# Expert weights as whole row blocks, rates by tiles, and two transfers' waits on other engines

## The reference, cut to what matters

```python
N, D, E, F = (4608, 512, 8, 1024)
logits = x @ w_gate
e_idx = np.argmax(logits, axis=1)
for e in range(E):
    mask = e_idx == e
    h = np.maximum(x[mask] @ w1[e], 0.0)      # w1[e]: 512 x 1024
    ye = h @ w2[e]                            # w2[e]: 1024 x 512
    out[mask] = gate_w[mask, None] * eom[mask, e, None] * ye
```

## Time and profile before

| | |
|---|---|
| median of 3 runs | 1118.25 us (1117.03 to 1119.43) |
| profiled execution, its own time | 1117.23 us |
| its span | 1115.5 us |
| PE busy | 1050.9 us, 94% |
| DVE, ACT, POOL busy | 581.8, 394.3, 221.9 us |
| mean granted clock of PE | 0.977 of full speed |
| first slot's input transposes | 596.0 us after the span's start |

### The profile page before, as it was taken

How to read it: one execution, slowest core, us unless ns; L and a number is a source line. 1 busy time by engine, 2 the same in 40 slices (tenths; PEclk the granted TensorE clock), 3 DMA queues, 4 the chain that set the end, 5 groups by cost and what they waited for, 6 DMA issues and landing times.

```text
span 1115.5 us, 22675 instructions
## 1 busy us (share of the span) xinstructions
PE 1050.9 (94%) x6189; PEld 873.4 (78%) x6190; DVE 581.8 (52%) x1182; ACT 394.3 (35%) x725; POOL 221.9 (20%) x411
## 2 busy tenths in 40 slices
PE   4899999999999999999965999999999999999695
PEld 3688888888888888888844888888888888888584
DVE  6876767677676767676643434324343332342320
ACT  3443333443343443343421334323333432332321
POOL 2463211212121212121211111111111111111010
PEclk9899999999999999999986999999999999999898
DMA  7542132322122322222003343423334242232100
GB/s 231 185 155 61 55 75 75 75 69 73 49 74 75 76 69 50 70 75 58 20 20 102 118 136 122 135 78 112 113 94 127 82 140 60 81 125 65 29 29 29
DMA packets 57270, 96.71 MB, mean 87 GB/s; under 512 B 15758, under 2 KB 15886, under 8 KB 57232
## 3 DMA queue, kind: packets, MB, share of 16 engines
q1 hardware_dynamic: 47168, 75.60, 22.5%
q0 software_dynamic: 7968, 20.61, 6.2%
q10 hardware_dynamic: 2096, 0.04, 0.1%
HBM read 76.66 MB, written 20.60 MB: 87 GB/s over the span
## 4 chain that ended last, share of the span: by engine, by line
PE 91%; DVE 3%; issue 2%; DMA 2%; ACT 1%; POOL 0%; ACTq 0%; DVEq 0%; SPq 0%; POOLq 0%
PE Y_ps L436 38%; PE H_ps L436 36%; PE T L428 6%; PE S_ps L483 3%; PE X_ps L428 3%; PE X_ps L493 3%; PE S_ps L428 2%; PE L_ps L520 1%; DVE wx L707 1%; DMA stage<-in_moe_w_out 0%; DMA wg<-in_moe_w_output_gate 0%; DMA prob<-x_rows,slot_rec 0%; POOL route_table L1033 0%; DVE dl L707 0%; DVE cen L752 0%
## 5 line engine op out<-in xcount | busy, mean ns | idle before, releaser
L436 PE MATMUL Y_ps<-wx,dh 128*128 (+1 forms) x1216 | 386.1, 399 | 2.4 <-DVE dl L707 2.4
L436 PE MATMUL H_ps<-wx,xh 128*128 (+1 forms) x1216 | 337.2, 399 | 12.2 <-DVE wx L707 8.7
L436 PEld LDWEIGHTS H_ps<-wx,xh 128*128 128x128 f32 x1216 | 225.9, 191 | 56.5 <-issue 11.6
L436 PEld LDWEIGHTS Y_ps<-wx,dh 128*128 128x128 f32 x1216 | 220.1, 188 | 49.3 <-issue 8.1
L436 PE MATMUL Y_ps<-wx,dl 128*128 (+1 forms) x608 | 237.6, 391 | 0.0
L436 PE MATMUL H_ps<-wx,xl 128*128 (+1 forms) x608 | 188.8, 392 | 0.0
L707 DVE TENSOR_TENSOR wx<-stage,wx (+1 forms) x63 | 76.5, 1224 | 157.0 <-ACT wx L660 156.4
L436 PEld LDWEIGHTS H_ps<-wx,xl 128*128 128x128 f32 x608 | 115.0, 189 | 24.7
L436 PEld LDWEIGHTS Y_ps<-wx,dl 128*128 128x128 f32 x608 | 114.1, 188 | 24.8
L739 DVE TENSOR_REDUCE nmax_h<-H_ps 128x1 f32<-128x1024 f32 x36 | 44.1, 1224 | 90.1 <-PE H_ps L436 86.3
L1057 POOL DMA_INDIRECT out<-x,slot_rec x40 | 40.6, 1014 | 215.7 <-ACT x L685 203.7
(11 more groups left out here) (173 smaller groups left out, 1238.2 us busy)
## 6 DMA issues: line engine op xcount, KB each, us to landing
stage<-in_moe_w SPq DMA_DIRECT2D x128, 256.0 KB, 3.0
stage<-in_q SPq DMA_DIRECT2D x36, 256.0 KB, 2.9
stage<-in_k SPq DMA_DIRECT2D x72, 128.0 KB, 3.3
stage<-in_v SPq DMA_DIRECT2D x36, 256.0 KB, 3.2
x_rows<-x SPq DMA_DIRECT2D x36, 256.0 KB, 2.3
stage<-in_moe_w_out SPq DMA_DIRECT2D x4, 512.0 KB, 3.7
stage<-in_moe_w_in SPq DMA_DIRECT2D x3, 512.0 KB, 8.5
slot_rec<-route_table SPq DMA_DIRECT2D x40, 2.0 KB, 1.6
```

The source lines that it names most:

```text
L436: i = pe.matmul(acc[:, c0:c0 + HALF], x[:, kk, :], w(part, kk * cols + c0), start=first and x is hi and part == 0, stop=last and x is lo)
```

## The change

**Row blocks.** The host lays the weights out anew as one input `experts`: for each expert 8 blocks of 128 rows x 1024, first 4 row blocks of `w1`, then 4 pairs of row blocks of `w2`. A piece is one block, loaded by one DMA of 512 KB. H waits for an expert's first 4 pieces, and Y of the slot before waits for all 8 of its expert. Y also starts after the first half of `dl` (`g0_lo`) and waits for the second half (`g1_lo`) in its middle.

**Rates by tiles.** Pieces per slot are 2 for experts of 4 tiles or more, 4 for 2 or 3 tiles, 8 for 1. They reach `(idx + 0.5) * pace` in the middle and `(idx + 1) * pace` at the end of a slot. `i_load` becomes the table of the splits itself, so SP issues a load as soon as the piece 8 before it is split.

**Records by POOL, last waits on SP.** `load_rec` moves to POOL, and SP instead of POOL waits for the landing of the last scatters.

```diff
@@ tables written by DVE
-            link(dve.tensor_scalar(idx, idx, float(SPLIT_RATE), None, ALU.mult))
-            dve.tensor_scalar(mid, idx, float(PIECES), float(PIECES), ALU.min, ALU.add)
-            link(dve.tensor_scalar(idx, idx, 1.0, float(PIECES), ALU.add, ALU.min))
+            dve.tensor_scalar(rate, tiles, 3.5, 2.0, ALU.is_lt, ALU.mult)
+            link(dve.tensor_scalar(rate1, tiles, 1.5, 4.0, ALU.is_lt, ALU.mult))
+            link(dve.scalar_tensor_tensor(rate, rate, 2.0, rate1, ALU.add, ALU.add))
+            link(dve.tensor_tensor(rate1[:, 0:NE - 1], rate[:, 1:], rate[:, 0:NE - 1], ALU.subtract))
+            link(dve.tensor_tensor(wide1[:, :, 0:NE - 1], past[:, :, 0:NE - 1], rate1[:, 0:NE - 1].unsqueeze(1).to_broadcast([1, SLOTS, NE - 1]), ALU.mult))
+            link(dve.tensor_reduce(pace, wide1[:, :, 0:NE - 1], AX.X, ALU.add))
+            link(dve.tensor_scalar(pace, pace, rate[:, 0:1], None, ALU.add))
+            dve.tensor_tensor(mid, idx, pace, ALU.mult)
+            link(dve.scalar_tensor_tensor(idx, idx, 1.0, pace, ALU.add, ALU.mult))
+            link(dve.scalar_tensor_tensor(mid, pace, 0.5, mid, ALU.mult, ALU.add))
+            dve.tensor_scalar(idx, idx, float(PIECES), None, ALU.min)
+            link(dve.tensor_scalar(mid, mid, float(PIECES), float(PIECES), ALU.min, ALU.add))
...
-            link(dve.tensor_scalar(least[:, 0:SLOTS], mid, float(-PIECES), None, ALU.add))
-            link(dve.tensor_tensor(least, least, first, ALU.max))
-            link(dve.tensor_tensor(least, least, till, ALU.min))
             dve.tensor_copy(i_split[:, :], till)
-            dve.tensor_scalar(i_load[:, :], least, limit8, None, ALU.min).then_inc(slots_set, 1)
+            dve.tensor_scalar(i_load[:, :], till, limit8, None, ALU.min).then_inc(slots_set, 1)
@@ SP
-                sp.dma_start(buf[:, 0, :], w1r[bass.ds(row1, P), bass.ds(i % 2 * PW, PW)]).then_inc(raw_in, 16)
-                sp.dma_start(buf[:, 1, :], w2r[bass.ds(row2, P), :]).then_inc(raw_in, 16)
+                sp.dma_start(to, experts[bass.ds(row, P), :]).then_inc(raw_in, 16)
...
-                if has(3):
-                    if has(-1):
-
-                        sp.wait_ge(out_st[(u + 3) % 4], uses(c, u - 1, 4) * 16)
-                    load_rec(c, u + 3)
...
-            slot_steps(sp, slot)
+            last = slot_steps(sp, slot)
+            for b in range(4):
+                wait_alone(sp, out_st[b], last * 16 + 16, passed)
@@ PE
-                    pe.wait_ge(split, at * PIECES + PIECES)
+                    pe.wait_ge(split, at * PIECES + KD)
...
-                    pe.wait_ge(g0_lo, s); pe.wait_ge(g1_lo, s)
+                    pe.wait_ge(split, before * PIECES + PIECES)
+                    pe.wait_ge(g0_lo, s)
                     at_least(pe, y_ev, s - 1)
                     for kk in range(KF):
+                        if kk == KF // 2:
+                            pe.wait_ge(g1_lo, s)
@@ POOL
+            def load_rec(c, u):
+
+                base = pool.value_load(i_base[0:1, bass.ds(c * 4 + u, 1)], min_val=0, max_val=TROWS - P)
+                pool.dma_start(slot_rec[u % 4][:, :], table[bass.ds(base, P), :]).then_inc(rec_in[u % 4], 16)
...
+                if has(3):
+                    if has(-1):
+                        wait_alone(pool, out_st[(u + 3) % 4], uses(c, u - 1, 4) * 16, passed)
+                    load_rec(c, u + 3)
+            pool.wait_ge(bases_set, 1)
+            pool.wait_ge(rec_st, 16 * NT)
+            for i in range(2):
+                load_rec(0, i)
             gather(0, 0)
-            last = slot_steps(pool, slot)
-            for b in range(4):
-                wait_alone(pool, out_st[b], last * 16 + 16, passed)
+            slot_steps(pool, slot)
```

More of the change, by code:

```diff
@@ L28 @@
 RING = 8
-SPLIT_RATE = 2
-LOAD_RATE = 2
 def at_least(eng, sem, count):
@@ L51, in uses, with build @@
     return c * (4 // ring) + k // ring + 1
-def build(nc, q, k, v, w_in, w_out, g_ln, w_gate, w_ogate, w1, w2, out):
+def build(nc, q, k, v, w_in, w_out, g_ln, w_gate, w_ogate, experts, out):
     f32, f32r, i32, u32 = mybir.dt.float32, mybir.dt.float32r, mybir.dt.int32, mybir.dt.uint32
@@ L265, in build, with first_at @@
         HOME = (0, 1, 2, 3, 2, 3, 2, 3)
[L267 to L269 removed]
+        def first_at(part, i, buf=1):
+            return wx[:, buf, part, i // KD, i % KD * FF:(i % KD + 1) * FF].rearrange("p (l n) -> p l n", l=2)
         def wts(buf, part, layer, c0, n):
@@ L289, in split_pieces @@
                     eng.wait_ge(ready, (p + 1) * each)
-                    cols = bass.ds(p % PIECES * PW, PW)
+                    cols = bass.ds(p % PIECES * 2 * PW, 2 * PW)
                     buf = bass.ds(p // PIECES % 2, 1)
-                    flat = "p b l n -> p (b l) n"
-                    part(stage[:, bass.ds(p % RING, 1), :, :].rearrange(flat),
-                         wx[:, buf, 0, :, cols].rearrange(flat), wx[:, buf, 1, :, cols].rearrange(flat))
+                    both = wx[:, :, :, :, :].rearrange("p b t l n -> p b t (l n)")
+                    part(stage[:, bass.ds(p % RING, 1), :, :].rearrange("p b l n -> p (b l n)"),
+                         both[:, buf, 0, cols].rearrange("p b n -> p (b n)"), both[:, buf, 1, cols].rearrange("p b n -> p (b n)"))
         def halves(T):
@@ L323, in load_first, with load_raw0 @@
                     sp.dma_start(to, rows.rearrange("(l p) n -> p l n", l=2)).then_inc(done, 16)
[L325 to L337, removed]
+            def load_raw0(p):
+                to = raw[:, p % 2, :, :].rearrange("p l n -> p (l n)")
+                sp.dma_start(to, experts[p * P:(p + 1) * P, :]).then_inc(raw0_in[p % 2], 16)
             load_qk(0, 0, 0)
@@ L411, in slot @@
                             wait_alone(sp, split, p + 1, passed)
-                            wait_alone(sp, raw_in, (p + RING) * 32, passed)
+                            wait_alone(sp, raw_in, (p + RING) * 16, passed)
                             load_raw(p + RING)
-            for s in range(2):
-                load_rec(0, s)
             sp.wait_ge(slots_set, 1)
-            sp.sem_inc(raw_in, PIECES * 32)
-            slot_steps(sp, slot)
+            sp.sem_inc(raw_in, PIECES * 16)
+            last = slot_steps(sp, slot)
+            for b in range(4):
+                wait_alone(sp, out_st[b], last * 16 + 16, passed)
         @block.tensor
@@ L677, in slot @@
                 if has(0):
-                    split_pieces(act, *mid, raw_in, 32, high)
+                    split_pieces(act, *mid, raw_in, 16, high)
                 if has(-1):
@@ L687, in slot @@
                 if has(0) or has(1):
-                    split_pieces(act, *end, raw_in, 32, high)
+                    split_pieces(act, *end, raw_in, 16, high)
             act.wait_ge(slots_set, 1)
@@ L870, in _ @@
             tiles, ends, gap, act1, rank, zero = (temp(NE) for _ in range(6))
+            rate, rate1 = temp(NE), temp(NE)
             past, wide1, below = (temp(SLOTS * NE).rearrange("o (j e) -> o j e", e=NE) for _ in range(3))
-            n_past, base, idx, kk, mid, own = (temp(SLOTS) for _ in range(6))
-            till, first, least = (temp(SLOTS + 1) for _ in range(3))
+            n_past, base, idx, kk, mid, own, pace = (temp(SLOTS) for _ in range(7))
+            till = temp(SLOTS + 1)
             limit, limit8 = temp(1), temp(1)
@@ L989, in split_piece @@
             def split_piece(src, buf, i, p):
-                cols = bass.ds(i * PW, PW)
-                hi, lo = wx[:, buf, 0, :, cols], wx[:, buf, 1, :, cols]
+                hi, lo = (first_at(part, i, buf) for part in range(2))
                 pool.tensor_copy(hi, src).then_inc(split_hi, 1)
@@ L1077 @@
         laid[name] = inputs[name].reshape(UN, 2, H, NCH, CH, D).transpose(order).reshape(NT * P, H * CH)
+    first = inputs["moe2_w1"].reshape(NE, KD, P, FF)
+    second = inputs["moe2_w2"].reshape(NE, KD, 2, P, DM).transpose(0, 1, 3, 2, 4).reshape(NE, KD, P, FF)
+    laid["experts"] = np.concatenate([first, second], axis=1).reshape(NE * PIECES * P, FF)
     for name in _INS:
```

24 lines of the change are left out of this document (6 added, 18 removed).

## The result

| | before | after |
|---|---|---|
| median | 1118.84 us (1117.03 to 1119.52, 4 runs) | 1100.01 us (1099.93 to 1100.83, 4 runs) |
| ratio | | 0.984, interval 0.9828 to 0.9851 |
| profiled execution, span | 1117.23, 1115.5 us | 1100.04, 1098.4 us |
| mean granted clock of PE | 0.977 | 0.986 |

What follows compares the result with a forecast made beforehand. PE was taken as the bound (busy 1050.9 of 1115.5 us), so only its idle time and the end could be won. -10.6 - 0.6 - 1.9 + 1.0 = -12.1 on 1117.2, plus 1.0 for the median: 1106.1 us, range 1103.0 to 1110.5.

Steps and rivals of the forecast that it cites:

- step 3: Block's end: with the last waits off POOL, its drain starts earlier at unchanged length; -1.9 us, at most 2.7.
- Step 4: Handoff between the stages: records fetched by POOL land later and the gather overlaps weight loads; +1.0 us, from 0 to +5.8.
- The range's lower end: Forecast time of 1103.0 us: drain gains 2.7, handoff costs 0, and the runs' spread of 1.2 us lies below.
- Step 1: Boundary at expert 7: PE's 8.7 us wait for weight pieces goes, and 1.86 us of low clock with it; -10.6 us.
- The cover: Slot end: `dl` is ready 1.8 us before Y starts; a second piece takes 1.15, 0.6 remain, so no cost.
- Step 2: Last slot: Y starts on the first half of `dl`, ready one subtraction earlier; -0.6 us.
- The rival of POOL's chain: Slots: POOL's scatter-fetch-gather chain, with 4.8 us of room, becomes the bound and the kernel slower, 1124 us; chance 0.04.
- Step 5: Costed at nothing: one 512 KB DMA for two, more loads at once at slot starts, the first stage's pieces on POOL.
- The step from the profile to the median: Whole kernel: the runs' median lies 1.0 us above the profiled execution, so 1105.1 becomes 1106.1 us.

Runs made afterwards that it cites:

- experiment 1: Kernel before, with only the last four waits for landings on SP in place of POOL: 1116.25 us, ratio 0.998.
- 5: Kernel after, with records fetched by SP and the old pacing of SP's loads put back: 1104.37 us, ratio 0.9881.
- 9: Kernel before with the last waits on SP, plus a dummy 2 KB fetch by POOL in all 40 slots: 1112.37 us, ratio 0.9945.
- experiment 2: Kernel after, with only the last four waits for landings back on POOL: 1101.77 us, ratio 0.9852.
- experiment 3: Kernel after, with one rate, two pieces split per slot for every expert: 1104.34 us, ratio 0.987.
- experiment 8: Kernel after, with Y waiting for both halves of `dl` at its start: 1102.77 us, ratio 0.987.
- experiment 4: Kernel after, with the records fetched by SP; last waits on SP, row blocks and rates kept: 1116.74 us, ratio 0.9987.
- experiment 11: Kernel before with the last waits on SP, plus a dummy 2 KB POOL fetch in three of four slots: 1118.95 us, ratio 1.0004.
- 7: Kernel before with the last waits on SP, plus one dummy 2 KB fetch by POOL in slot 3: 1118.02 us, ratio 1.0.
- 12: Kernel after, plus a dummy fetch by POOL in each of the 40 slots: 1103.49 us, ratio 0.9872.
- 6: Kernel before with the last waits on SP, plus one dummy 2 KB POOL fetch just ahead of the last scatter: 1117.64 us, ratio 0.9997.
- 9 to 12: Dummy POOL fetches added to experiment 1 in all, every fourth, three of four slots; to kernel after in all: 1112.37, 1117.68, 1118.95, 1103.49 us.

## Why the prediction was wrong

**The step that failed** is the term of step 3 in the sum: "POOL's drain starts at 1108.6, after the landing, and takes 6.61 us". The prediction moved the start of a drain of fixed length, -1.9. The mechanism and its size hold where the drain's length is kept: 1.9 in experiment 1. But in the change POOL also issues 40 DMAs more, and with 165 in place of 125 the drain needs 1.54 us in place of 6.61. Measured for the end: -6.0 = -1.9 (waits) - 4.1 (count; experiments 5 and 9 give it alone: 7.8 to 3.7 behind, 7.8 to 3.8). Taken in the other order, by experiment 2, the count brings 5.1 and the waits 0.9. Step 4 listed what 40 fetches cost in the handoff and in the slots and nothing at the block's end, where they counted most. The range's lower end had the same gap: it gave the drain at most 2.7.

The prediction asked whether the drain's 6.61 us are what the Trainium skill has for a first call of freshly loaded POOL code ("GPSIMD Engine Reference", section "Instruction dispatch": about 6 us). The page says nothing of drains, and the reading does not hold here: for the same instruction at the same place, 1.54 to 9.06 us were measured, by the number of DMAs. Another page of the Trainium skill, "VectorE: DVE Perf Modes", section "The DRAIN you can't avoid", has the drains at a kernel's edges constant at about 12 ns on all engines. Of the block's end here only SP's is near that, 7 ns in the kernel after; ACT's takes 0.72 us, DVE's 0.92, PE's 3.67 and POOL's 3.75. The Trainium skill's "DMA: Bandwidth & Descriptors", section "Terms", says that DMAs of POOL go by descriptors which software writes into rings. No run here shows whether the drain has to do with these rings; why its length goes with the count stays open.

**Step 1, the boundary:** -10.6 forecast, -10.8 measured, by the mechanism given; 5.7 of the wait went by the row blocks and the start half a slot earlier, 3.05 by the rates (experiment 3). The cover at the end of slot 34's pieces shrank from 1.8 to 0.7 us, as forecast (0.6).

**Step 2, Y on half of `dl`:** -0.6 forecast and measured (2.01 to 1.41), 0.8 in experiment 8.

**Step 4, the handoff:** +1.0 forecast, +0.3 measured. The landing of the first fetch was right, 2.2 us at most (590.20 to the gather at 592.39). What was counted too dear is the way there: POOL starts its fetch 0.2 us after SP did, and issues the gather 2.2 us later, where before 2.5 us lay between SP's fetch and POOL's gather (590.01 to 592.52). The gather's overlap with the weight loads came out at nothing: 3.5 us from the gather's issue at 592.39 to PE at 595.90, the same as before. In the slots the gather is issued 9.6 us before its transposes (1020.93 to 1030.52), 10.2 before the change. The rival of POOL's chain had room to the end. The Trainium skill gives simple loads to SP and calls its kind of DMA generally faster ("DMA: Bandwidth & Descriptors", section "Issuing engine by pattern"). The trace agrees: the landings have a median of 2.6 us in place of 1.6. In the slots that costs nothing since all of it is hidden.

**Step 5, costed at nothing:** right for the kernel as a whole, but experiment 4 shows what it hung on. The loads at once at the start of the slots are harmless only because the records no longer stand behind them on SP; apart from POOL's fetches they cost 12.4 us (1116.74 - 1104.37).

**The step from the profile to the median:** +1.0, and 0 measured (1100.01 against 1100.04 profiled). In the profiled executions of the seven kernels that keep the 8.7 us gap, the time from the first input transposes to the last Y spread from 501.8 (experiment 11) to 504.4 us (7), in four without a gap behind the first slot (after, 2, 5 and 12) only from 491.3 (12) to 491.8 (2). Some of the scatter that the 1.0 stood for may have gone with the gap; one execution of each kernel doesn't show it.

By the profile the miss is 17.1 - 12.1 = 5.0 us: 4.1 of the drain, 0.7 of the handoff, 0.4 of the first stage, 0.2 at the boundary, less the 0.4 of the first slot. The missing 1.0 of the median makes it 6.1.

## What to carry to other kernels

Look at the instructions behind the last product as at any other: how long POOL's last drain takes and what it follows is worth as much as a stall, and an edit that gives POOL more or fewer DMAs may move it by microseconds either way. When a transfer is moved to another queue, ask what it stood behind there: the move may be what lets another part of the same change go well. A gap of PE can cost its length and then some clock, also when it is short: 1.9 us more in the one profiled execution with a gap of 3.05 us, while two other runs of that kernel show no such loss in their mean clock. So price the clock behind a gap as a range, and look at more than one execution.

## What the runs showed of the hardware that was not expected

- POOL's drain at the block's end takes 6.6, 6.7, 7.4 and 9.1 us after 125, 126, 135 and 155 DMAs of POOL, 1.54 after 165 and 5.1 after 205. Where between 156 and 165 it falls, and whether it goes by DMAs or by their descriptors, stays open.
- In the profiled execution of experiment 3, with 3.05 us without work for PE ending at 1043.10, the granted clock was 0.85 in the window from 1040 to 1045 and 0.81 in the next. The slot behind a gap is not of fixed length: behind the same 8.7 us it took 13.85 (11) to 15.16 us (7) in seven profiled executions, where an ordinary one takes 12.24.
- In kernels 6 and 7 the 16-byte buffer of the dummy fetch lay ahead of other buffers in SBUF and moved them by 16 bytes per partition. Their ordinary slots took 12.27 us in place of 12.24. In 9 to 12 the buffers lay at the end, and slots took 12.24. Whether the placement does it is not shown: both profiled executions were the slowest of ten of their kernel (1120.83 us where the lowest was 1116.51, and 1121.36 where it was 1116.40), and no faster one was profiled.
